# Loading the second-layer weights in 4 KB rows, with the hidden units in another order

## The reference, cut to what matters

```python
# x: (2, 11456, 128), inducing: (32, 128), w1: (8, 128, 1024), w2: (8, 1024, 128), fp32
h   = mab(inducing, x)        # mab(q, kv) = softmax(q @ kv.T / sqrt(128)) @ kv
att = mab(x, h)               # 22912 points of 128
def moe(x, logits, w1, w2):   # once with cosine logits / tau, once with x @ w_gate + bias[modality]
    e    = argmax(logits); gate = softmax(logits)[e]
    return gate * (relu(x @ w1[e]) @ w2[e])
out = moe(moe(att, ..., w1a, w2a), ..., w1b, w2b)
```

## Time and profile before

| | |
|---|---|
| time, median of 3 runs (lowest to highest) | 1064.76 us (1063.57 to 1066.66) |
| the profiled execution: its time, its span | 1066.66 us, 1064.9 us |
| PE busy, share of the span | 982.6 us, 92% |
| DVE, ACT, POOL busy | 759.4, 672.7, 202.8 us |
| DMA queue q1: packets, MB, share of 16 engines | 66505, 70.41 MB, 21.3% |

### The profile page before, as it was taken

One profiled execution on the slowest core, in us unless ns is written; L12 is line 12 of the kernel. 1 busy time (PEld: TensorE's weight loads), 2 busy tenths in 40 slices (PEclk: granted clock), 3 DMA queues, 4 the chain that ended last, 5 costly groups with the idle time before them and its releaser, 6 DMA issues.

```text
span 1064.9 us, 27216 instructions
## 1 busy us (share of the span) xinstructions
PE 982.6 (92%) x6367; PEld 496.1 (47%) x6367; DVE 759.4 (71%) x2221; ACT 672.7 (63%) x1622; POOL 202.8 (19%) x437
## 2 busy tenths in 40 slices
PE   7677827999999999999999999999999999999886
PEld 5454312454444545445444454444444444444443
DVE  5675945677786777867778677786777867778554
ACT  5553723566666666666666666666666666666553
POOL 6870011111111111111111111111111111111100
PEclk9886958899999999999999999999999999999999
DMA  9995711001101011010110101101011010110000
GB/s 339 387 393 185 237 31 33 26 24 39 34 24 49 24 39 34 24 49 24 39 34 24 49 24 39 34 24 49 24 40 33 24 49 25 40 32 24 18 22 21
DMA packets 66552, 70.99 MB, mean 67 GB/s; under 512 B 33326, under 2 KB 55638, under 8 KB 65225
## 3 DMA queue, kind: packets, MB, share of 16 engines
q1 hardware_dynamic: 66505, 70.41, 21.3%
HBM read 40.81 MB, written 23.55 MB: 60 GB/s over the span
## 4 chain that ended last, share of the span: by engine, by line
PE 86%; DMA 5%; DVE 4%; issue 3%; ACT 2%; POOL 0%; SPq 0%; ACTq 0%; DVEq 0%; POOLq 0%
PE y L1295 45%; PE up L1318 23%; PE up L1308 7%; DMA GW<-in_x 3%; PE y L1372 2%; PE up L1234 1%; PE TB L1334 1%; PE TB L1358 1%; PE SM L1346 1%; DMA wraw<-in_moe_w 1%; PE SM L1366 1%; DVE GW L728 1%; PE up L1155 1%; DVE hlo L878 1%; DMA E4T<-E 1%
## 5 line engine op out<-in xcount | busy, mean ns | idle before, releaser
L878 DVE SCALAR_TENSOR_TENSOR hlo<-up,hhi 128x500 f16<-128x500 f32 x736 | 493.9, 672 | 170.7 <-ACT hhi L606 168.0
L606 ACT ACTIVATE hhi<-up 128x500 f16<-128x500 f32 x736 | 424.2, 583 | 170.3 <-PE up L1318 84.2
L1318 PE MATMUL up<-ytb,W1B 128*128 (+1 forms) x1104 | 276.1, 380 | 11.9 <-issue 11.6
L1295 PE MATMUL y<-hhi,W2A 128*128 128x500 f16 x736 | 218.2, 378 | 10.5 <-DVE hlo L878 5.5
L1295 PE MATMUL y<-hhi,GW 128*128 128x500 f16 x736 | 214.9, 373 | 0.4 <-DVE hlo L878 0.4
L1318 PEld LDWEIGHTS up<-ytb,W1B 128*128 x1104 | 108.6, 99 | 148.5 <-issue 39.7
L1308 PE MATMUL up<-E4T,GW 128*128 (+1 forms) x368 | 139.4, 382 | 0.0
L1295 PE MATMUL y<-hlo,W2A 128*128 128x500 f16 x368 | 138.8, 377 | 0.0
L1295 PE MATMUL y<-hlo,GW 128*128 128x500 f16 x368 | 137.4, 373 | 0.0
L1295 PEld LDWEIGHTS y<-hhi,W2A 128*128 x736 | 68.2, 98 | 93.1 <-issue 46.2
L516 POOL TENSOR_TENSOR st<-ss,root 125x4 f32<-125x4 f32 x46 | 46.8, 1018 | 250.8 <-ACT TB L632 250.8
(11 more groups left out here) (164 smaller groups left out, 1021.0 us busy)
## 6 DMA issues: line engine op xcount, KB each, us to landing
wraw<-in_moe_w SPq DMA_DIRECT2D x24, 512.0 KB, 5.0
xth<-x_turned SPq DMA_DIRECT2D x46, 250.0 KB, 2.8
out<-yout SPq DMA_DIRECT2D x46, 250.0 KB
GW<-in_x SPq DMA_DIRECT2D x10, 1024.0 KB, 10.2
x_turned<-GW SPq DMA_DIRECT2D x10, 1000.0 KB, 9.4
W1B<-in_moe_w SPq DMA_DIRECT2D x8, 512.0 KB, 11.5
x_turned<-GW SPq DMA_DIRECT2D x2, 750.0 KB, 7.0
GW<-in_x SPq DMA_DIRECT2D x1, 768.0 KB, 10.0
```

Of the source, the lines that this page charges most:

```text
L606: nc.scalar.activation(hhi[:, (u % UP) * CT:(u % UP + 1) * CT], ups[u % UP][:, 0:CT], ACT.Relu).then_inc(s["hi_done"], 1)
L878: nc.vector.scalar_tensor_tensor(hlo[:, o:o + CT], ups[u % UP][:, 0:CT], 0.0, hhi[:, o:o + CT], ALU.max, ALU.subtract).then_inc(s["lo_done ...
L1295: ins = mm(y[:, 0:CT], W[:, bass.ds(woff + (fb * 2 * C + o), C)], h[:, k * CT:(k + 1) * CT], start=opens and fb == 0 and n == 0, stop=fb = ...
L1318: ins = mm(ups[k][:, 0:CT], W1B[:, bass.ds(woff + (wl * F + fb * P), P)], ytb[:, bass.ds(yoff + yl * CW, CT)], start=n == 0, stop=n == 2)
```

## The change

The rows of w2 are dealt to partitions in another order: partition p takes the eight rows p\*8 to p\*8+7, which lie behind one another in DRAM. So every load of a w2 moves one run of 4096 bytes per partition where it moved eight runs of 512 bytes. Block f of the hidden units is now the units p\*8+f for all p. To match, whatever splits w1 reads every eighth column: for `W1B` from `wraw` in SBUF (in `high_low`, kind "w1"), for `G` from the product in PSUM (ACT and DVE). The targets `W1B` and `tmp16` are written in runs of 128 and 512 elements as before or packed; `G` is written in eight runs of 64. The number and the order of instructions stay on every engine.

```diff
@@ high_low (kind "w1": source of the split of w1b)
-                        a.rearrange("p (f c) -> p f c", f=NF))
+                        a.rearrange("p (c f) -> p f c", f=NF))
@@ load_w2a (8 loads)
-                sp.dma_start(w2raw[:, e, :].rearrange("p (f c) -> p f c", c=C), w2a[e, :, :].rearrange("(f p) c -> p f c", p=P)).then_inc(
+                sp.dma_start(w2raw[:, e, :], w2a[e, :, :].rearrange("(p f) c -> p (f c)", p=P)).then_inc(
@@ load of w2b (8 loads)
-                sp.dma_start(w2s[:, e % 2, :].rearrange("p (f c) -> p f c", c=C), w2b[e, :, :].rearrange("(f p) c -> p f c", p=P)).then_inc(
+                sp.dma_start(w2s[:, e % 2, :], w2b[e, :, :].rearrange("(p f) c -> p (f c)", p=P)).then_inc(
@@ ACT, copies of the products of G
-                    hi, product = tmp16[:, k % 3, :], gbank(k)[:, :]
+                    hi = tmp16[:, k % 3, :].rearrange("p (f c) -> p f c", f=NF)
+                    product = gbank(k)[:, :].rearrange("p (c f) -> p f c", f=NF)
@@ DVE, writes of G
-                    o = G[:, (b * NE + e) * F + q * 512:(b * NE + e) * F + (q + 1) * 512]
-                    hi, product = tmp16[:, k % 3, :], gbank(k)[:, :]
+                    o = G[:, (b * NE + e) * F:(b * NE + e + 1) * F].rearrange("p (f c) -> p f c", f=NF)
+                    o = o[:, :, q * (P // 2):(q + 1) * (P // 2)]
+                    hi = tmp16[:, k % 3, :].rearrange("p (f c) -> p f c", f=NF)
+                    product = gbank(k)[:, :].rearrange("p (c f) -> p f c", f=NF)
```

## The result

| | before | changed |
|---|---|---|
| time, median of 4 runs (lowest to highest) | 1064.16 us (1062.96 to 1066.66) | 1072.16 us (1071.90 to 1075.10) |
| ratio to before, 95% interval | | 1.0079 [1.0059, 1.0098] |
| the profiled execution: its time, its span | 1066.66, 1064.9 us | 1073.95, 1072.2 us |
| DVE's bias of the last quad (end of the first stage) | 88.16 us | 99.05 us |
| first scores of the third stage on PE (end of the second) | 136.27 us | 147.34 us |

The forecast was 1060.0 us in a range of 1057.3 to 1070.0.

What follows compares the result with a forecast made beforehand. It took DMA to bound the first stage, DVE the second and PE the third, from 138 us on. Savings of 3.2+1.6 = 4.8 us took the median from 1064.76 to 1060.0 us, range 1057.3 to 1070.

Steps and rivals of the forecast that it cites:

- by that nearest row ACT's and the SBUF ones too: Splits of w1: strided reads on ACT and from SBUF cost nothing, judged by the PSUM read at L819.
- My upper ends: Splits of w1b from SBUF: time per element doubled, +1.06 us per split on DVE, +0.85 us on ACT.
- My own sign of being wrong: Splits of w1: any of four durations (L552 1067, L734 1200 to 1600, products 596 and 744 ns) grown 40% or more.
- Rival two: Splits of w1b: strided reads of SBUF alone are slow; 1062.9 us or about 1069; chance 0.12.
- Its cheaper case: Rival on slow SBUF reads, only DVE's part counting: compute pace 7.2 us per quad, time 1062.9 us; whole rival 0.12.
- the rival's dearer case: Rival on slow SBUF reads, ACT's part also in series: pace 8.0 us, time about 1069; whole rival 0.12.
- The DMA term, 3.2 us: First stage: eight w2a loads each 0.4 us shorter, saving 3.2 us, bounds 1.4 to 4.6.
- so the time saved on each moves the following landings forward: First stage: with full engines, all eight w2a loads bring later landings of points forward, 8*0.4 = 3.2 us.
- The five dips of the earlier trace: First stage: DMA rate drops to 323 to 349 GB/s, one per quad's w2a, taken to show 0.4 us per load.
- A term beside it that I had put at nothing: First stage: SP may be free sooner with fewer packets to queue; costed at nothing, as transfer order stays.
- The second stage, 1.6 us: Shorter w2b transfers bring w1a forward, four longer steps each give back 0.4 us: 1.6 us, bounds 0 and 2.6.
- The third stage: From 138 us on: PE's limit, instructions and tiles untouched, so carried over unchanged.

Runs made afterwards that it cites:

- layer a alone: The full change, but with w2b's loads and the split of w1b as in the kernel before: 1062.84 us against 1064.70, ratio 0.9975 [0.9953, 0.9998].

## Why the prediction was wrong

The result fell outside the range on the slow side, and the way was wrong.

**The step that failed: "by that nearest row ACT's and the SBUF ones too" cost nothing.** From one read of PSUM with a gap (L819) I went to reads of SBUF. The row was right for what it showed: the 64 reads of PSUM cost nothing. SBUF is another memory, no row showed such a read, and I carried the value over where I should have kept it open. The size per split is +1.03 us on ACT and +0.83 us on DVE (1.20 to 2.03 us where nothing else delays it). My upper ends were 0.85 and 1.06 us: right in their sum, 1.91 against the 1.86 measured. Eight splits put 8\*1.86 = 14.9 us in series, and 10.0 and 12.8 us of it showed in the first stage, where I had written nothing. My own sign of being wrong came with it: L552 grew by 96%.

**Rival two was what happened.** It had 0.12 of the chance and two prices: 1062.9 us if only DVE's part counts and about 1069 us with ACT's part in series. Both count. With DVE or ACT alone the chip gave 1066.25 and 1065.95 us; with both 1072.16. I had put the pace with both at 8.0 us a quad; it was 8.6 in the first profile, and (82.12-32.56)/6 = 8.3 in the second. The result is still above the rival's 1069. That number takes off 1.2 us for three early quads and 1.6 us for the second stage, and neither came, as shown below; without them it is about 1071.8. (Its cheaper case has a slip: 0.2 us in each of five quads are 1.0 us and not 1.2.) That the rival's dearer case lay just inside my range, and its chance at 0.12 in total, is a second error: a rule that says every such read pays, with no row against it for SBUF, deserved more than one chance in eight.

**The DMA term, 3.2 us, was right in its mechanism and too large.** The rate rose as worked out, from 395 to 417 GB/s. The four kernels without a step of 16 B in the split ended the first stage at 87.55, 86.23, 85.73 and 86.14 us, 86.4 in the mean, against 88.16 and 88.96: 2.1 us. The part that failed is "so the time saved on each moves the following landings forward", for all eight w2a loads. PE first waits for points at quad 4. The load of quad 4 is issued only when quad 0 is mixed, at 18 us; what the first three w2a, which stand ahead of it, saved before that became idle DMA. The five dips of the earlier trace rows fit the other five. These are the windows of the first 20 us, kernel before, and then layer a alone:

```profile
0.00:20.00 20.00, 15.20 (x134) 12.54 (x135) 9.10 (x20) 9.77 (x21) 11.38 (x46) 1.00 0.88 319
```

```profile
0.00:20.00 20.00, 15.22 (x132) 12.53 (x133) 9.27 (x19) 9.56 (x20) 12.47 (x47) 1.00 0.81 304
```

The DMA share fell from 0.88 to 0.81 and PE did the same work. PE's first stall ended at 28.77 us with layer a alone and at 28.96 and 27.79 in the two profiles of before, so nothing had been gained by then; at quad 9, behind the other five, it was the 2.4 us above. Five loads at 0.4 us are 2.0 us, which is about what is left. That it is these three loads is read from the traces and was not tried by itself.

A term beside it that I had put at nothing was not nothing: SP. An issue of w1b right behind a w2a in 512 B rows held SP for 4.07 to 6.64 us in 18 to 56 us of the kernel before, and 0.43 to 0.56 us with layer a alone. The first of them, before and then with layer a alone:

```profile
18.95 6.64 SPq L329 DMA_DIRECT2D wraw<-in_moe_w  x1
```

```profile
19.18 0.46 SPq L329 DMA_DIRECT2D wraw<-in_moe_w  x1
```

The load of quad 5 was issued at 23.35 us instead of 26.11. How much of the 2.4 us comes from earlier issues and how much from faster packets no run here separates. The packets' own durations between 20 and 70 us (28.9 ns in the mean for 512 B, 162 ns for 4 KB) give 1.85 and 1.30 us a load, so they alone would be enough.

**The second stage, 1.6 us, was nearly nothing.** The median from issue to landing of the loads in 104 to 145 us was 4.6 us before and 4.2 in the changed kernel, but also 4.2 in the second profile of before and 4.1 with layer a alone, both with w2b in 512 B rows; so that w1a lands sooner is not shown. The seven steps between the remainders of w2b took 28.98, 28.50 and 28.73 us with rows of 512 B and, leaving out the two profiles with the fallen clock (31.29 and 31.02), 28.13, 27.88, 28.71, 28.27, 28.74, 28.88, 29.37 and 28.16 with 4 KB: 0.2 us less in the mean, which is nothing against their spread. With the two it is 0.3 us more. The steps of 3.77 us, DVE's pace, are there in every profile, and so are longer ones with a wait for a load. (The 34.3 us that I took for eight experts of now was also too high: the first two steps are 3.77 us as well, and the seven take 28.98.)

**The third stage** was right to be carried over, but its spread of 5 us from one profile to the next is larger than every term of my sum.

## What to carry to other kernels

A rearrangement that makes a transfer contiguous often makes some engine's read strided; before trading, look up in the trace how long that operation is, which engine waits for it, and in which memory it reads. A step of 16 bytes or more over SBUF made an fp32 operation take about 2 times as long on ACT and 1.6 to 1.7 times on DVE here, a step of 8 did not, and an fp16 write with a step of 256 bytes was worse than either; the gather with a step of 32 bytes out of PSUM was free, so do it where the data leaves PSUM. And time saved on DMA counts only from the first transfer that somebody waits for.

## What the runs showed of the hardware that I had not expected

- SBUF, fp32 source, 1024 elements per partition: ACT 1.06 us at a step of 4 B, 1.13 at 8, 2.04 at 16, 1.98 to 2.09 from 32 to 512. DVE 1.23 at 8, 1.92 to 2.35 from 16 on, beside 1.20 at least without a step.
- PSUM, fp32 source with a step of 32 B, 512 elements: ACT 596 ns and DVE 743 ns, as without a step.
- Writes of fp16 to SBUF with a step of 256 B, 1024 elements: ACT 4787 ns against 1067. DVE, which also read its fp16 operand so, 5033 ns.
- PE's weight load of 128x128 fp16 with a step of 16 B: 145 ns against 99, almost all of it hidden.
